# Local attention on 64-query sub-tiles: quadrant score products, a ones column in V, denominators applied after the attention product

## The reference, cut to what matters

```python
# q, k, v: (2, 8, 768, 64), float32
block, window = 32, 16
k_sum = k.reshape(B, H, nb, block, D).max(axis=3)        # nb = 24 block summaries
v_sum = v.reshape(B, H, nb, block, D).mean(axis=3)
scores_l = scale * (q @ k^T), kept where |i - j| < window, else -1e9
scores_s = scale * (q @ k_sum^T) + log(block)
a = softmax over [scores_l, scores_s]                    # e / (sum(e) + 1e-9)
attn = a @ [v, v_sum]                                    # (2, 8, 768, 64) -> x (1536, 512)
# first layer: h = x @ w_in (512 x 1024); solu = h * softmax(h); layer norm; @ w_out
# second layer: elu(x @ w2_in) @ w2_out, hidden width 2048
```

## Time and profile before

| | us |
|---|---|
| Median of 3 runs | 561.48 (559.33 to 562.39) |
| Profiled execution, its span | 555.4 |
| First unit's scores taken by DVE | 13.65 |
| Last unit's score product, second pass | 133.3 |
| First product of the first layer | 134.78 |

### The profile page before, as it was taken

One profiled execution on the slowest core, in us unless ns is written; L12 is line 12 of the kernel. 1 busy time (PEld: TensorE's weight loads), 2 busy tenths in 40 slices (PEclk: granted clock), 3 DMA queues, 4 the chain that ended last, 5 costly groups with the idle time before them and its releaser, 6 DMA issues.

```text
span 555.4 us, 7904 instructions
## 1 busy us (share of the span) xinstructions
PE 517.8 (93%) x2736; PEld 450.5 (81%) x2736; DVE 299.5 (54%) x837; ACT 241.8 (44%) x569; POOL 112.9 (20%) x113
## 2 busy tenths in 40 slices
PE   4787887879999999999999999999999999999997
PEld 2565665657888989889999998998998998998996
DVE  7999999997467264355346333333333333333332
ACT  2666675766366264345465443322223222232222
POOL 5443426250001100202338762000000000000000
PEclk9989999989999999999999999999999999999999
DMA  9997755402400000008000000100001000010001
GB/s 200 184 218 162 176 130 122 116 1 99 206 1 1 0 1 0 1 1 303 1 0 1 1 0 1 57 1 2 0 0 57 0 0 0 0 57 0 0 0 58
DMA packets 50751, 29.96 MB, mean 54 GB/s; under 512 B 44704, under 2 KB 44704, under 8 KB 49824
## 3 DMA queue, kind: packets, MB, share of 16 engines
q1 hardware_dynamic: 50720, 29.57, 20.2%
HBM read 25.83 MB, written 3.15 MB: 52 GB/s over the span
## 4 chain that ended last, share of the span: by engine, by line
PE 76%; DVE 14%; issue 5%; ACT 2%; DMA 1%; POOL 1%; SPq 0%; DVEq 0%
PE bank L878 11%; PE bank L880 11%; PE bank L879 11%; PE bank L1049 8%; PE bank L1050 8%; PE bank L1048 8%; PE bank L1006 3%; PE bank L1008 3%; PE bank L1007 3%; DVE se L700 3%; DVE se L714 2%; DVE rc L708 2%; PE bank L914 2%; PE bank L992 2%; DMA vblocks<-in_v 1%
## 5 line engine op out<-in xcount | busy, mean ns | idle before, releaser
L854 DVE TENSOR_SCALAR ex<-ex 128x384 f32<-128x384 f32 x64 | 25.3, 396 | 119.8 <-ACT ex L623 119.8
L880 PE MATMUL bank<-yt_lo,w2in_hi 128*128 (+1 forms) x256 | 86.3, 337 | 0.0
L878 PE MATMUL bank<-yt_hi,w2in_hi 128*128 (+1 forms) x256 | 86.2, 337 | 0.0
L879 PE MATMUL bank<-yt_hi,w2in_lo 128*128 (+1 forms) x256 | 86.0, 336 | 0.0
L623 ACT ACTIVATE ex<-bank 128x384 f32<-128x384 f32 x64 | 31.5, 491 | 119.9 <-PE bank L880 119.9
L1050 PE MATMUL bank<-w2out_hi,g_lo 128*128 128x512 f32 x192 | 76.0, 396 | 0.0
L1049 PE MATMUL bank<-w2out_lo,g_hi 128*128 128x512 f32 x192 | 75.8, 395 | 0.0
L1048 PE MATMUL bank<-w2out_hi,g_hi 128*128 128x512 f32 x192 | 74.6, 389 | 0.0
L861 DVE TENSOR_TENSOR g_lo<-gf,g_hi 128x384 fp32r<-128x384 f32 x64 | 38.7, 605 | 41.5 <-ACT g_hi L631 41.5
L506 ACT ACTIVATE se<-se,nm 128x192 f32<-128x192 f32 x96 | 42.8, 447 | 38.9 <-DVE nm L700 38.6
L631 ACT ACTIVATE g_hi<-gf 128x384 fp32r<-128x384 f32 x64 | 33.6, 525 | 58.9 <-DVE gf L858 58.7
(11 more groups left out here) (107 smaller groups left out, 964.6 us busy)
## 6 DMA issues: line engine op xcount, KB each, us to landing
w2in_raw<-in_w_in SPq DMA_DIRECT2D x1, 4096.0 KB, 12.9
w2out_raw<-in_w_out SPq DMA_DIRECT2D x4, 1024.0 KB, 9.5
kraw<-in_k SPq DMA_DIRECT2D x16, 192.0 KB, 3.4
qraw<-in_q SPq DMA_DIRECT2D x16, 192.0 KB, 3.9
vblocks<-in_v SPq DMA_DIRECT2D x4, 768.0 KB, 6.5
va<-in_v SPq DMA_DIRECT2D x16, 192.0 KB, 3.3
out<-osb SPq DMA_DIRECT2D x12, 256.0 KB, 2.1
win_raw<-in_w_in SPq DMA_DIRECT2D x4, 512.0 KB, 5.2
```

The source lines that it names most:

```text
L878: pe.matmul(acc, ah, bh, start=(i == 0), stop=False)
L879: pe.matmul(acc, al, bh, start=False, stop=False)
L880: last = pe.matmul(acc, ah, bl, start=False, stop=(i == n - 1))
```

## The change

A unit is still 128 queries of two heads, but each half of it (64 queries) now sees its own 96 local keys (64 and 16 on each side) and the 24 summaries, 120 columns for each head.

- `kt` holds the transposed k of a pair once, with 16 zero columns at each end; a sub-tile's window is a slice of it. The copies of POOL (`windows`) and of the maxima (L687) are gone, and ACT copies k with one instruction of 128 partitions. DVE takes the block maxima from `kt`.
- `scores` is four products of 64 x 64 (depth 64, 64 queries) into 96 columns, and four into 24 columns, each in its own quadrant; the two heads write different banks.
- DVE masks 120 columns a head instead of 192; the exponentials are 120 wide, without a sum.
- `turn_probs` is two transposes; their PSUM tile is now single.
- V lies as `vw`: 120 rows for each sub-tile and head, 64 columns and a column of ones. `attend` is four products of depth 120, 64 queries and 65 columns into one tile `psO`, queries on the partitions; column 64 is the denominator.
- Every three units DVE adds 1e-9 to the six denominators, inverts them and scales the output out of PSUM (`normalise`); PE transposes the result (`turn_x`, three transposes); `copy_x` and `low_x` follow. The last step comes six or seven units behind instead of three or four.
- Tiles m = 0 and m = 1 of the first layer now both stand in the attention's tail.

```diff
+    SUB = P // 2
+    SUBS = S // SUB
+    LOCAL = SUB + 2 * HALO
+    KEYS = LOCAL + NB
+    D1 = D + 1
...
-        psS = [bank(0), bank(1)]
-        psP = [bank(2), bank(3)]
-        psO = [bank(4), bank(5)]
+        psS = [[bank(0), bank(1)], [bank(2), bank(3)]]
+        psP = bank(4)
+        psO = bank(5)
         psQK = banks[3]
+        psX = [bank(6), bank(7)]
...
-        T_LAG, PV_LAG = 2, 3
+        T_LAG, PV_LAG, X_LAG = 2, 3, 6
...
+                    rows = vf[2 * n + h].rearrange("(j i) d -> i j d", i=SUB)
+                    sp.dma_start(vw[HALO:HALO + SUB, s, :, h, 0:D], rows).then_inc(v_loaded[s], 16)
+                    sp.dma_start(vw[0:HALO, s, 1:SUBS, h, 0:D],
+                                 rows[SUB - HALO:SUB, 0:SUBS - 1, :]).then_inc(v_loaded[s], 16)
+                    sp.dma_start(vw[HALO + SUB:LOCAL, s, 0:SUBS - 1, h, 0:D],
+                                 rows[0:HALO, 1:SUBS, :]).then_inc(v_loaded[s], 16)
...
-            def windows(n):
...
-                    last = act.activation(se[:, s, cols], se[:, s, cols], ACT.Exp, scale=-1.0,
-                                          bias=nm[:, s, h:h + 1], accum_out=ss[:, s, h:h + 1])
+                    last = act.activation(se[:, s, h, :], se[:, s, h, :], ACT.Exp, scale=-1.0, bias=nm[:, s, h:h + 1])
...
-            def normalise(u):
-                s = u % RING
-                dve.wait_ge(expd, u + 1)
-                dve.tensor_scalar(rc[:, s, :], ss[:, s, :], 1e-9, None, ALU.add).then_inc(denom_added, 1)
-                dve.wait_ge(denom_added, u + 1)
-                dve.reciprocal(rc[:, s, :], rc[:, s, :]).then_inc(recip_ready, 1)
-                dve.wait_ge(recip_ready, u + 1)
-                for h in range(2):
-                    cols = slice(h * KEYS, (h + 1) * KEYS)
-                    last = dve.tensor_scalar(se[:, s, cols], se[:, s, cols], rc[:, s, h:h + 1], None, ALU.mult)
-                last.then_inc(probs_ready, 1)
...
+            def normalise(w):
+
+                heads = psO[:, 0:2 * TG * D1].rearrange("p (i c) -> p i c", c=D1)
+                dve.wait_ge(attn_done, TG * (w + 1))
+                dve.tensor_scalar(rs[:, w % 2, :], heads[:, :, D], 1e-9, None, ALU.add).then_inc(denom_added, 1)
+                dve.wait_ge(denom_added, w + 1)
+                dve.reciprocal(rc[:, w % 2, :], rs[:, w % 2, :]).then_inc(recip_ready, 1)
+                dve.wait_ge(recip_ready, w + 1)
+                if w >= 2:
+                    dve.wait_ge(x_in_psum, w - 1)
+                dve.tensor_tensor(xn[:, w % 2, :, :].rearrange("p t (h d) -> p (t h) d", h=2), heads[:, :, 0:D],
+                                  rc[:, w % 2, :, None].broadcast_to([P, 2 * TG, D]), ALU.mult).then_inc(xn_ready, 1)
...
-                pe.matmul(psS[u % 2][:, 0:2 * KEYS], qt[:, s, t * P:(t + 1) * P], kw[:, s, t, :],
-                          start=True, stop=True).then_inc(scores_in_psum, 1)
+                for i in range(2):
+                    j = 2 * t + i
+                    for h in range(2):
+                        rows = slice(h * D, (h + 1) * D)
+                        pe.matmul(psS[u % 2][h][i * SUB:(i + 1) * SUB, 0:LOCAL], qt[rows, s, j * SUB:(j + 1) * SUB],
+                                  kt[rows, s, j * SUB:j * SUB + LOCAL], start=True, stop=True)
+                if t == 0:
+                    pe.wait_ge(ks_ready, n + 1)
+                for i in range(2):
+                    j = 2 * t + i
+                    for h in range(2):
+                        rows = slice(h * D, (h + 1) * D)
+                        last = pe.matmul(psS[u % 2][h][i * SUB:(i + 1) * SUB, LOCAL:KEYS],
+                                         qt[rows, s, j * SUB:(j + 1) * SUB], ks[rows, s, :], start=True, stop=True)
+                last.then_inc(scores_in_psum, 1)
...
+                pe.wait_ge(expd, u + 1)
+                if u >= 1:
+                    pe.wait_ge(*pt_copied(u - 1))
+                pe.transpose(psP[0:KEYS, 0:P], se[:, s, 0, :], ident[:, :])
+                pe.transpose(psP[0:KEYS, P:2 * P], se[:, s, 1, :], ident[:, :]).then_inc(probs_in_psum, 1)
...
+                if u % TG == 0 and w >= 1:
+                    pe.wait_ge(xn_ready, w)
+                for h in range(2):
+                    c0 = (u % TG * 2 + h) * D1
+                    for i in range(2):
+                        q0 = h * P + i * SUB
+                        last = pe.matmul(psO[i * SUB:(i + 1) * SUB, c0:c0 + D1], pt[0:KEYS, u % 2, q0:q0 + SUB],
+                                         vw[0:KEYS, v, 2 * t + i, h, :], start=True, stop=True)
+                last.then_inc(attn_done, 1)
+
+            def turn_x(w):
+                pe.wait_ge(xn_ready, w + 1)
...
+                for t in range(TG):
+                    last = pe.transpose(psX[w % 2][:, t * P:(t + 1) * P], xn[:, w % 2, t, :], ident[:, :])
+                last.then_inc(x_in_psum, 1)
...
-                if UNITS <= u < UNITS + 2:
-                    rows_product(0, u - UNITS)
+                if UNITS <= u < UNITS + 4:
+                    rows_product((u - UNITS) // 2, (u - UNITS) % 2)
```

More of the change, by code:

```diff
@@ L388, in _ @@
-            for first, width, base, sign in regions:
-                m = mask[:, 1, first:first + width]
-                last = pool.affine_select(out=m, in_=m, compare_op=ALU.is_ge, fill=NEG, base=base,
-                                          pattern=[[sign, width]], channel_multiplier=-sign)
-            step(last)
-            for h in range(2):
-                m = mask[:, 1, 2 * h * P:(2 * h + 1) * P]
-                pool.affine_select(out=m, in_=m, compare_op=ALU.is_ge, fill=NEG, base=WINDOW - 1,
-                                   pattern=[[-1, P]], channel_multiplier=1)
-                summary = KA + h * KB + 2 * HALO
-                pool.memset(mask[:, 1, summary:summary + NB], LOG_BLOCK / SCALE)
-                last = pool.memset(mask[:, 1, summary + NB:KA + (h + 1) * KB], NEG)
@@ new lines, in _ @@
+            for half, offset in ((0, 0), (1, SUB)):
+                m = bands[:, half, :]
+                step(pool.affine_select(out=m, in_=m, compare_op=ALU.is_ge, fill=NEG, base=offset - 1,
+                                        pattern=[[1, LOCAL]], channel_multiplier=-1))
+                step(pool.affine_select(out=m, in_=m, compare_op=ALU.is_ge, fill=NEG, base=2 * WINDOW - 1 - offset,
+                                        pattern=[[-1, LOCAL]], channel_multiplier=1))
+            step(pool.memset(mask[:, :, LOCAL:KEYS], LOG_BLOCK / SCALE))
@@ L478, in _, with copy_k @@
         def _(act):
-            def copy_kv(n):
-                s = n % 2
-                act.wait_ge(kmax_ready, n + 1)
-                if n == 0:
-                    act.wait_ge(consts_ready, 2)
-                if n == 1:
-                    act.wait_ge(consts_ready, 4)
+            def copy_k(n):
+                act.wait_ge(kv_in_psum, n + 1)
                 if n >= 2:
                     act.wait_ge(scores_in_psum, T * (n - 1))
-                for h in range(2):
-                    rows = slice(h * D, (h + 1) * D)
-                    last = act.activation(kw[rows, s, :, 2 * h * P:(2 * h + 1) * P],
-                                          psQK[rows, 0:S].rearrange("p (t c) -> p t c", t=T), ACT.Copy)
-                last.then_inc(kv_copied, 1)
+                act.activation(kt[:, n % 2, HALO:HALO + S], psQK[:, 0:S], ACT.Copy).then_inc(kt_ready, 1)
             def copy_q(n):
@@ L513, in copy_pt @@
                     act.wait_ge(attn_done, u - 1)
-                act.activation(pt[:, u % 2, :], psP[u % 2][:, 0:3 * P], ACT.Copy).then_inc(pt_by_act, 1)
+                act.activation(pt[0:KEYS, u % 2, :], psP[0:KEYS, 0:2 * P], ACT.Copy).then_inc(pt_by_act, 1)
             def copy_x(w):
-                act.wait_ge(attn_done, TG * (w + 1))
+                act.wait_ge(x_in_psum, w + 1)
                 act.activation(xt_hi[:, w // HALVES, (w % HALVES) * GT:(w % HALVES + 1) * GT],
-                               psO[w % 2][:, 0:GT], ACT.Copy).then_inc(xhi_ready, 1)
-            copy_kv(0)
+                               psX[w % 2][:, 0:GT], ACT.Copy).then_inc(xhi_ready, 1)
+            copy_k(0)
             copy_q(0)
-            for u in range(UNITS + PV_LAG):
+            for u in range(UNITS + X_LAG):
                 n, t = u // T, u % T
@@ L725, in low_x @@
                 dve.wait_ge(xhi_ready, w + 1)
-                dve.tensor_tensor(xt_lo[:, n, cols], psO[w % 2][:, 0:GT], xt_hi[:, n, cols].bitcast(F32),
+                dve.tensor_tensor(xt_lo[:, n, cols], psX[w % 2][:, 0:GT], xt_hi[:, n, cols].bitcast(F32),
                                   ALU.subtract).then_inc(xlo_ready, 1)
-            pair_prep(0)
-            dve.wait_ge(consts_ready, 3)
-            for kind, halo in ((0, 0), (2, HALO)):
-                step(dve.tensor_copy(mask[:, kind, :], mask[:, 1, :]))
-                for h in range(2):
-                    first = KA + h * KB + halo
```

(9 more changed lines are left out.)

193 lines of the change are left out of this document (73 added, 120 removed).

## The result

| | before | after |
|---|---|---|
| Median of the runs, us | 561.32 (559.33 to 562.39, 4 runs) | 539.75 (535.73 to 541.32, 4 runs) |
| Ratio of the times, 95% interval | | 0.963 (0.957 to 0.969) |
| Profiled execution, its span | 555.4 | 533.9 |
| First unit's scores taken by DVE | 13.6 | 14.5 |
| Last unit's scores taken by DVE | 133.8 | 106.4 |

The changed kernel takes 21.6 us less. Medians, ranges and ratios here leave out a run more than 1.5% above the fastest of its kernel; that is one run of `e12_rows_tail` (549.48) and one of `e13_rows_tail_means` (544.00). By the spans, the difference of 21.5 us splits so: the start +0.9; the stage from the first to the last score 120.2 to 91.9, -28.3; from there to tile m = 2, 14.9 to 19.1, +4.2; the rest 406.7 to 408.4, +1.7.

What follows compares the result with a forecast made beforehand. DVE, with waits for POOL, was taken to pace the attention stage, PE right behind. PE's terms summed to 2.30 us a unit, -9.2; +1.7 at the start and +3.6 at the tail made -3.9: 557.5 us, range 532 to 588.

Steps and rivals of the forecast that it cites:

- rival A: Faster: PE's different quadrants overlap in weight loads too, other limits hold a unit at about 1.85 us; 536 us, chance 0.26.
- the signs that were to show the forecast wrong: PE waiting for DVE or ACT in most units, or the clock row having more than the two falls of before.
- The 25 us that the prediction counts as waiting for POOL: DVE's scaling L714 losing 17.6 us and its addition L708 7.8 us in the attention stage, against undisturbed times.
- the prediction's sentence on the reciprocal: After the change, no DVE operation on the path but the reciprocal reads and writes only SBUF, so no stalls behind POOL.
- The score term of the sum: PE's 16 score passes a unit, loads one behind the other, 0.91 us; bounds 0.22 (all four quadrants at once) and 1.8.
- The changes of shape: PE switching array shape between scores, transposes and attention product: 0.10 us each, 3.33 a unit, 0.33 us a unit.
- Rival B: Slower: each change of shape empties PE's array and shows its load, 0.26 us; 2.84 a unit, 583 us, chance 0.26.
- Rival C: Slower: PE's small passes cost as much as one of 128 columns, 0.11 us; 3.6 a unit, about 620, chance 0.06.
- Rival D: Slower: PE's clock falls to 0.50 and stays; a unit costs 4 us, about 640 us in all, chance 0.06.
- The transfers: 168 KB more a pair for V's neighbours and means, 0.8 us at 212 GB/s, hidden by the later pairs.
- The term of +1.7 at the start: PE at half clock until about 17 us now sets the pace at the stage's start, costing +1.7 us.
- The tail: PE loses its cover for the 4.1 us before tile m = 2; less saved transposes, +3.6 us.

Runs made afterwards that it cites:

- e12_rows_tail: Changed kernel with tile m = 1 behind the last turn_x and k and q loaded in packets of 1536 bytes instead of 256: 533.33 us, ratio 0.953.
- e13_rows_tail_means: As e12_rows_tail, with the next pair's block means also placed ahead of the weights: 532.66 us, ratio 0.956 to the kernel before.
- e4_before_no_norm: Kernel before without its normalise (addition, reciprocal and scaling left out, output not divided): 529.07 us in one run, against 557.93.
- e6_before_pool_copies: Kernel before with POOL's eight subtractions (remainders of w_in and w_out) replaced by copies: 547.74 us, ratio 0.981.
- e3_short_loads: Changed kernel loading only a sixth of k and q from pair 2, and of V's own rows from pair 3: 523.96 us in one run.
- e14_one_row_half: Changed kernel with both heads' score products on rows 0 to 63, only two quadrants used: 589.37 us in one run, against 558.64 for the kernel before.
- e1_tail: Changed kernel with tile m = 1 of the first layer back behind the last turn_x: 531.48 us, ratio 0.950 to the kernel before.
- e0_changed: The changed kernel run again, unaltered, beside its variants: 537.31 us, ratio 0.962 to the kernel before.
- e2_wout_late: Changed kernel with the four loads of w_out (2 MB) issued behind the last pair's loads: 535.39 us, ratio 0.959 to the kernel before.
- e8_means_first: Changed kernel with the next pair's block means placed ahead of the weights: 535.31 us, ratio 0.961 to the kernel before.

## Why the prediction came out as it did

The forecast was 557.5 with 532 to 588 around it, and faster at 0.47. The measured 539.75 lies in the range but 7 us below the forecast's own 547 to 568. It lies in the range because rival A does, given 536 and a chance of 0.26; the sum itself had the scores and the attention product wrong, and the transfers. Of the signs that were to show the forecast wrong neither came: PE waits for DVE or ACT in few units, and the clock has two falls, though one of 20.5 us. PE is 88% busy, just under the nine tenths.

**DVE and POOL: right, shown.** DVE set the pace through its `normalise`, and L714's waits for POOL were part of that (`e4_before_no_norm`, `e6_before_pool_copies`). The 25 us that the prediction counts as waiting for POOL are there: the 18 long operations are 24.9 us over their medians, 15.0 of it behind the subtractions. `e6_before_pool_copies` takes 1.3 us off each of the eight and gains 10.2; the waits for POOL's other operations have no run of their own. DVE's work after was predicted at 62 us and is 51; ACT, bounded by 79.4, is 56.8. No operation of DVE in the stage is longer than 0.94 us. That one, the block maxima, now also reads and writes only SBUF, which the prediction's sentence on the reciprocal leaves out.

**The score term of the sum: the step that failed.** It took the weight loads one behind the other, 16 x 0.057 = 0.91; with a change that is 1.01 us, and 0.41 was measured. The attention product, with "two halves at once" as its lower bound, was put at 0.46 and a change, 0.56, and took 0.38. The loads of different quadrants overlap, as the two blocks at the half clock show, 0.68 on four and 1.26 on two. A unit's own work with its three changes was 1.89 in the sum and is 1.15, so PE needs 0.74 us a unit less than forecast. The range's lower bound had the right case; I took the value in the middle, though the row it rested on, two loads 0.06 apart, shows full-array loads and says nothing of quadrants. The Trainium skill, TensorEngine Tiling (Array Packing), section Tiling Modes, says that different tiles can execute loads and products in parallel; the runs agree (0.68 against 1.26), and here it should have weighed more than that row.

**The changes of shape: right in size.** The last transpose to the first attention product is 0.20 us (67.14 to 67.34) where transposes follow at 0.11 (67.03 to 67.14), 0.09 for the change; it was taken at 0.10. Rival B's 0.26 is not seen anywhere. By the same section of the Trainium skill, a change of the tiling mode drains the engine; whatever it does inside, the trace prices it at a tenth of a microsecond.

**A wait put at nothing.** The sum had 0.05 us a unit for the single `psP` and weighed `psO`. It had nothing for the banks that `psX` now shares with the transposes of q: 0.82 us a pair, 0.14 a unit, wherever nothing else holds the stage (`e3_short_loads`).

**Rival C** doesn't fit: 16 small score passes take 0.41 us with a change, not 16 x 0.11. **Rival D** came in part. The clock fell for 20.5 us of the stage and came back, which cost an estimated 7.8 us as worked out above. In `e14_one_row_half` it was low for the whole stage.

**The transfers: the second step that failed.** The prediction had the later pairs hide the added bytes, since the stage moved at 129 GB/s on average. But a stage that is a quarter shorter must move the same loads faster: 16.96 MB from 14 to 106 us, at 184 GB/s, with a share near 1 up to 94 us and not only until 54. At 1.54 us a unit PE would be through in 74 us; the stage took 18 us more. Rival A held its unit at 1.85 by "the loop over DVE, ACT and `psP`" and the early DMA. Measured are 1.91, and 1.69 in a pair, 1.67 over the stage, once the loads are short: for about 0.2 us a unit the transfers, with the fall of the clock behind them, are the cause. It comes to more than that in pairs 1 and 2 and to little in the others. Which limit of the transfers it is stays open.

**Where the gain of the new products went.** It was lost to this. The old products without `normalise` end the stage at 105.9, with the clock at 1.00 from 17.1 us on; the new ones end it at 106.4, with 20.5 us at 0.50. The gain of this change is DVE's `normalise` taken off the path. The cheaper products did pay where the loads were light: a stage of 80.2 us.

**Both ends.** The term of +1.7 at the start was for PE at the half clock until 17 us. It ran there until 24.2 us; 9.7 us of the stage at 1.92 us a unit against 1.15 are an estimated 3.9, and this lies in the stage's 91.9. The +0.9 of the table is another thing, the first score itself coming later, and was not in the sum. The tail was put at +3.6: the wait is 4.16, the stretch +4.2, the mechanism as described, and `e1_tail` gives 5.8 back. Not in the sum was the half clock behind the wait, 1.7 us, though the earlier trace rows had shown such a fall.

The sum again with what was measured: +0.9 for the first score, -28.3 for the stage (forecast -9.2 and +1.7), +4.2 and +1.7 for the tail, -21.5.

## What to carry to other kernels

When the engine that sets the pace is relieved, price the loads at the new, shorter stage (its bytes over its length, and the queue that issues them) before counting a second engine's saving as gain. The vector engine's scaling from SBUF to SBUF, 0.32 us by its median, took up to 2.3 beside subtractions on the general engine; look at an operation's largest duration against its median. When two uses are put into the same PSUM banks, price the wait of one for the other. Where a stage's last step has a chain of small operations behind it, keep a piece of independent work for PE there: it saved the wait and the slow clock after it.

## What the runs showed of the hardware that was not expected

- Sixteen float32 passes over 64x64 quadrants (eight of 96 columns, eight of 24), their weight loads and a change of shape take 0.41 us at full clock, little more than the 0.32 between the two passes of one product of 384 columns and a change.
- The clock fell to 0.50 for 20.5 us, and PE was busy for 19.5 of them. The fall came inside a wait of 1.48 us for k. Of the ten falls in the stages of `e0_changed`, `e1_tail`, `e2_wout_late` and `e8_means_first`, eight begin inside or within 0.1 us of PE's wait of 0.9 us or more for k or the means, and two 0.9 and 1.5 us behind one. With the score products on two quadrants only, a whole stage of 143 us ran at that level, by the distance of its transposes, although PE hardly paused (19.20 of 19.20 us busy). No run shows why.
- The profile's column of the clock reads 1.00 ahead of its first record even where transposes follow each other at twice their usual distance; the distances are the safer reading.
